# Attention's score maxima in eleven pieces instead of fifteen, the short query tile over either half of the keys

## The chip, the cores and the metric

The kernel runs on one core of one Trainium2 chip. The metric is the device time of one execution in microseconds. The median of three runs of the kernel before is 1193.37 us (1192.91 to 1196.4).

## The reference, cut to what matters

```python
def _attn_ref(q, k, v):                       # q, k, v: (4, 8, 1152, 64)
    q_pool = q.reshape(B, H, S // 2, 2, D).mean(axis=3)          # 576 queries
    scores = scale * np.matmul(q_pool, k.transpose(0, 1, 3, 2))  # 576 x 1152
    scores = scores - np.max(scores, axis=-1, keepdims=True)
    attn = np.exp(scores)
    attn = attn / (np.sum(attn, axis=-1, keepdims=True) + 1e-09)
    return np.matmul(attn, v)
```

The 32 heads (4 batches of 8) of this attention come first. A mixture of four attention experts with a top-2 gate, a low-rank mix over the sequence and a wide two-layer network follow; the change touches none of them.

## The kernel before, in words

The program has three parts, `attention`, `experts` and `mlp`. In `attention` each engine has its own list of instructions, written out by hand in Python loops over the heads; nothing plans it, and an engine goes strictly through its list. Semaphores order the engines against each other.

A head has 576 pooled queries in five tiles of 128 (`QT`; the last, the *short tile*, holds 64, `LAST`, and 64 columns of zeros) and 1152 keys in nine tiles (`KT`). Its scores are computed twice on TensorE:

- Once with the queries on the partitions, to find each query's maximum. This is the work of `max_piece`. Each of its matmuls has a tile of 128 queries as stationary operand and a third of the keys (`PIECE`, 384 columns) moving, and fills one of two banks, `maxes[0]` and `maxes[1]`, in turn. VectorE reduces the bank to one value a partition (L647) and so frees it (`max_freed`). Five tiles by three thirds make 15 pieces a head, in the order of `PIECES`.
- Once with the keys on the partitions (`score`, nine a head, four matmuls of 288 columns each: two at L392, two at L401, which also subtract the maxima, carried by the transposed `q_lo_m`). ScalarE takes the exponential (L576, `exponent`), TensorE multiplies with the values (`values`, L415), and GpSimd (`add_tiles`, L264 and L270) and VectorE (`add_late`, L668 and L673, and `sum_blocks`, L679 and L681) add the exponentials up.

The work of two heads is interleaved: while the scores of head h run, the pieces of head h + 1 fill the gaps between them. TensorE's list for a head is, before the change: score 0, pieces 0 and 1, the turning (transposing) of the last keys together with the short query tile, score 1, piece 2, score 2, piece 3, the turning of the queries of h + 2, piece 4, score 3, piece 5, the turning of the output of head h - 1 (`turn_out`, L426), piece 6, the row sums of head h - 1 (`sum_rows`, L431), piece 7, score 4, piece 8, the values of four tiles, pieces 9 and 10, score 5, piece 11, the turning of four key tiles of h + 2, piece 12, score 6, piece 13, score 7, piece 14, score 8, the turning of four more key tiles, the turning of the queries' low parts and maxima of h + 1 (`turn_q_lo_m`), the values of the other five tiles.

What holds TensorE: a piece waits until the piece two before it has been reduced; score n waits for exponential n - 2; `turn_q_lo_m` waits for the head's final maximum (`maximum`, L661), which reduces the partial ones in `part_max`. ScalarE's list has nine exponentials a head, and between them the copies out of PSUM (L546 and L547: the short query tile and the last keys; L550: four key tiles; L555: the queries; L562: low parts and maxima; L584: the output). VectorE's list: the 15 reductions of head h + 1 with `normalise(h - 1)` (L688 to L708) in front of the tenth, then L661, then the sums of head h, whose second step waits for GpSimd's additions. GpSimd's list holds, for each head, the low parts of keys and queries (L237, L246), a copy of the keys (L255), the pooling (L231) and six additions; in heads 8 to 14 it also splits the weights of the experts. The first head's maxima are computed apart (`wide_maxima`), with 1152 columns in three banks.

Of the kernel before, what the change touches and what calls it, by code (L numbers as in the profile page):

```python
# [26 lines left out]
P = 128  # L27
BANK = 512
EPS = 1e-9
MASKED = -1000000000.0  # L30

# [22 lines left out]
def attention(nc, q, k, v, x_all, x_ready, ident, ident_r, ready, ahead):  # L54
# [29 lines left out]
    PIECES = ([(t, c) for c in range(2) for t in range(QT - 1)] + [(QT - 1, 0), (QT - 1, 1)]  # L84
              + [(t, 2) for t in range(QT)])
# [18 lines left out]
    with ctx:  # L104
# [16 lines left out]
        qT = [sb(f"qT{u}", [P, WIDE], F32R) for u in range(3)]  # L121
        qTm = [sb(f"qTm{u}", [P, WIDE], F32R) for u in range(2)]
        part_max = [sb(f"part_max{u}", [P, QT, 3]) for u in range(2)]
# [30 lines left out]
        wide_reduced = sem("wide_maxima_reduced")  # L154
        padded = sem("padding_written")
# [28 lines left out]
        PADS = 8  # L184
# [133 lines left out]
        def _(pe):  # L318
# [53 lines left out]
            def max_piece(h, at):  # L372
                u, (t, c) = h % 2, PIECES[at]
                n = max_no(h, at)
                if at == 0:
                    pe.wait_ge(qa_copied, h + 1)
                for first, name in (((0, 0), "ka"), ((0, 1), "kb"), ((QT - 1, 0), "kc")):
                    if (t, c) == first:
                        pe.wait_ge(turn_freed, keys_before[name, h] + 1)
                if n >= 2:  # L380
                    pe.wait_ge(max_freed[n % 2], n // 2)
                nc.tensor.matmul(maxes[n % 2][:, 0:PIECE], qT[h % 3][:, t * P:(t + 1) * P],  # L382
                                 kT[u][:, c * PIECE:(c + 1) * PIECE], start=True, stop=True
                                 ).then_inc(max_filled, 1)
# [63 lines left out]
            for h in range(HEADS - 1):  # L448
# [17 lines left out]
                maxima(5, 6)  # L466
                if h > 0:
                    turn_out(h - 1)
                maxima(6, 7)
                if h > 0:  # L470
                    sum_rows(h - 1)
                maxima(7, 8)
                score(h, 4)
                maxima(8, 9)
                values(h, range(EARLY))
                maxima(9, 11)
                score(h, 5)
                maxima(11, 12)
                if more2:
                    turn_keys(h + 2, "ka", range(0, 4))  # L480
                maxima(12, 13)
                score(h, 6)
                maxima(13, 14)
                score(h, 7)
                maxima(14, 15)
# [38 lines left out]
        def _(act):  # L524
# [17 lines left out]
            def copy_keys(h, name):  # L542
                u = h % 2
                act.wait_ge(turned, turn_no[name, h] + 1)
                if name == "kc":
                    nc.scalar.activation(qT[h % 3][:, 4 * P:WIDE], turn[:, P:2 * P], ACT.Copy)  # L546
                    ins = nc.scalar.activation(kT[u][:, 8 * P:S], turn[:, 0:P], ACT.Copy)  # L547
                else:
                    at = 0 if name == "ka" else 4 * P
                    ins = nc.scalar.activation(kT[u][:, at:at + 4 * P], turn[:, :], ACT.Copy)  # L550
                ins.then_inc(turn_freed, 1)
# [91 lines left out]
        def _(dve):  # L643
            def max_piece(h, at):
                u, (t, c), n = h % 2, PIECES[at], max_no(h, at)
                dve.wait_ge(max_filled, n + 1)
                nc.vector.tensor_reduce(part_max[u][:, t, c:c + 1], maxes[n % 2][:, 0:PIECE],  # L647
                                        AX.X, ALU.max).then_inc(max_freed[n % 2], 1)

            def wide_maxima(t):  # L650
                dve.wait_ge(wide_filled, t + 1)
                nc.vector.tensor_reduce(part_max[0][:, t, :], wide(t), AX.X, ALU.max
                                        ).then_inc(wide_reduced, 1)

            def maximum(h):
# [3 lines left out]
                else:  # L659
                    dve.wait_ge(max_freed[n % 2], n // 2 + 1)  # L660
# [55 lines left out]
            nc.vector.memset(oT[:, HALF + SHIFT:3 * P], 0.0).then_inc(padded, 1)  # L716
            nc.vector.memset(group_sums[:, SQ // BLOCK:], 0.0).then_inc(padded, 1)
# [17 lines left out]
            for h in range(HEADS - 1):  # L735
                for at in range(len(PIECES)):
                    if at == 9 and h > 0:
# [1123 lines left out]
```

## Time and profile before

| | us |
|---|---|
| median of three runs | 1193.37 |
| the profiled execution, its own time | 1195.76 |
| its span, first to last instruction | 1194.0 |
| PE busy | 1135.8 |
| DVE busy | 651.6 |
| ACT busy | 543.9 |
| POOL busy | 523.4 |
| L647, 465 reductions of the pieces, DVE | 250.6 |
| L382, 465 matmuls of the pieces, PE | 166.0 |

The profile is one execution. PE is TensorE's matmuls, PEld its weight loads, DVE VectorE, ACT ScalarE, POOL GpSimd. A matmul's record is longer than the time it keeps the array, since successive matmuls overlap; the distance from one start to the next is what it costs. The heads fill the span from about 20 to 507 us, the experts follow to about 780, and the wide network runs to the end.

### The profile page before, as it was taken

The page shows a single profiled execution, that of the slowest core. Times are in us where ns is not written, and L with a number is a line of the kernel's source. Part 1 is how long each engine was busy: PE and PEld are TensorE (multiplying, and loading weights), DVE is VectorE, ACT ScalarE, POOL GpSimd, SP SyncE. Part 2 cuts the span into 40 slices and gives each one's busy share as a digit, 9 for nine tenths or more (in the row PEclk, how much of TensorE's full clock was granted, in tenths as well). Part 3 has the DMA queues.
Part 4 walks back from the last instruction along what each step waited for, and adds up shares of the span by engine and source line. Part 5 has one row for each costly group of instructions (what it writes and reads, how often), then busy time and mean ns, then how long its engine had stood idle before and what let it go on. Part 6 is the DMA issues. An engine that isn't in the chain of part 4 may idle for free. (4 is left out here: it accounts for less than half of the span.)

```text
span 1194.0 us, 19539 instructions
## 1 busy us (share of the span) xinstructions
PE 1135.8 (95%) x7232; PEld 951.8 (80%) x7232; DVE 651.6 (55%) x1370; ACT 543.9 (46%) x1131; POOL 523.4 (44%) x560
## 2 busy tenths in 40 slices
PE   6999999989999999997899999789999999999998
PEld 5777777777777778786777777489898989899896
DVE  5888877877888888866556565553121212122120
ACT  4666666556666666546565656633110201111110
POOL 6888899998888888734333333300000000000000
PEclk9999999999999999998999999999999999999999
DMA  8222111221111221002001010142100001010000
GB/s 205 61 60 61 56 46 51 60 60 46 51 55 60 60 60 41 22 27 115 2 1 41 1 45 24 40 146 62 53 1 27 27 1 53 0 53 0 27 1 27
DMA packets 47559, 54.56 MB, mean 46 GB/s; under 512 B 10992, under 2 KB 29424, under 8 KB 46960
## 3 DMA queue, kind: packets, MB, share of 16 engines
q1 hardware_dynamic: 46864, 53.12, 14.4%
q8 instruction: 53, 0.87, 0.3%
q10 hardware_dynamic: 608, 0.30, 0.1%
q14 instruction: 34, 0.28, 0.1%
HBM read 43.97 MB, written 9.44 MB: 45 GB/s over the span
## 5 line engine op out<-in xcount | busy, mean ns | idle before, releaser
L647 DVE TENSOR_REDUCE part_max<-psA 128x1 f32<-128x384 f32 x465 | 250.6, 556 | 59.4 <-PE psA L382 36.7
L576 ACT ACTIVATE pT<-psA 128x576 f32<-128x576 f32 x288 | 187.9, 653 | 165.5 <-PE psA L401 156.4
L270 POOL TENSOR_TENSOR pT<-pT 128x576 f32<-128x576 f32 x157 | 225.3, 1435 | 26.2 <-ACT pT L576 4.3
L382 PE MATMUL psA<-kT,qT 128*128 128x384 f32 x465 | 166.0, 379 | 11.5 <-DVE part_max L647 11.1
L415 PE MATMUL psA<-pT,v_raw 128*64 128x288 f32 x1152 | 153.8, 412 | 0.0
L1770 ACT ACTIVATE hid_hi<-psC 128x384 fp32r<-128x384 f32 x96 | 47.2, 492 | 198.7 <-PE psC L1695 198.6
L392 PE MATMUL psA<-qT,kT 128*128 128x288 f32 x576 | 132.2, 311 | 0.0
L1789 DVE SCALAR_TENSOR_TENSOR hid_lo<-psC,hid_hi 128x384 fp32r<-128x384 f32 x96 | 53.5, 558 | 137.9 <-ACT hid_hi L1770 137.9
L401 PE MATMUL psA<-qTm,kT 128*128 128x288 f32 x576 | 123.0, 295 | 0.5 <-ACT qTm L562 0.5
L415 PEld LDWEIGHTS psA<-pT,v_raw 128*64 128x64 f32 x1152 | 77.0, 136 | 53.2 <-issue 6.4
L1711 PE MATMUL psC<-w_hi,hid_hi 128*128 128x512 f32 x288 | 113.5, 394 | 0.0
L392 PEld LDWEIGHTS psA<-qT,kT 128*128 128x128 f32 x576 | 98.4, 189 | 18.4 <-issue 14.0
L382 PEld LDWEIGHTS psA<-kT,qT 128*128 128x128 f32 x465 | 83.7, 189 | 36.5 <-DVE part_max L647 19.4
L1711 PE MATMUL psC<-w_hi,hid_lo 128*128 128x512 f32 x288 | 112.3, 390 | 0.0
L1711 PE MATMUL psC<-w_lo,hid_hi 128*128 128x512 f32 x288 | 112.2, 389 | 0.0
L401 PEld LDWEIGHTS psA<-qTm,kT 128*128 128x128 f32 x576 | 92.3, 188 | 0.7 <-issue 0.7
L1695 PE MATMUL psC<-uT_hi,w_hi 128*128 128x384 f32 x384 | 82.5, 337 | 1.7 <-DVE uT_lo L44 1.7
L1147 POOL TENSOR_SCALAR moe_probs<-moe_probs,moe_sum_inv,gate 128x128 f32<-128x128 f32 (+4 forms) x80 | 53.7, 671 | 66.0 <-DVE moe_sum_inv L1520 61.8
L1695 PE MATMUL psC<-uT_hi,w_lo 128*128 128x384 f32 x384 | 82.4, 337 | 0.0
L1695 PE MATMUL psC<-uT_lo,w_hi 128*128 128x384 f32 x384 | 82.4, 337 | 0.0
L1410 ACT ACTIVATE moe_probs<-psB,moe_neg_max 128x128 f32<-128x128 f32 (+4 forms) x80 | 45.6, 570 | 65.4 <-DVE moe_neg_max L1533 64.7
L1695 PEld LDWEIGHTS psC<-uT_hi,w_hi 128*128 128x128 f32 x384 | 68.1, 188 | 2.4 <-DVE uT_lo L44 2.0
(165 smaller groups left out, 1948.2 us busy)
## 6 DMA issues: line engine op xcount, KB each, us to landing
k_raw<-in_k SPq DMA_DIRECT2D x32, 288.0 KB, 2.9
v_raw<-in_v SPq DMA_DIRECT2D x32, 288.0 KB, 2.8
q_raw<-in_q SPq DMA_DIRECT2D x31, 256.0 KB, 3.3
w_raw<-in_moe_w_ch SPq DMA_DIRECT2D x1, 4096.0 KB, 12.3
u_rows<-x_all SPq DMA_DIRECT2D x16, 256.0 KB, 2.0
w_raw<-in_moe_w_ch SPq DMA_DIRECT2D x16, 256.0 KB, 2.6
u_first<-u_rows SPq DMA_DIRECT2D x3, 768.0 KB, 4.5
u_second<-u_rows SPq DMA_DIRECT2D x3, 768.0 KB, 4.7
```

Of the source, the lines that this page charges most:

```text
L270: nc.gpsimd.tensor_tensor(pT[:, KT, :], pT[:, KT, :], pT[:, j, :], ALU.add).then_inc(part_summed, 1)
L382: nc.tensor.matmul(maxes[n % 2][:, 0:PIECE], qT[h % 3][:, t * P:(t + 1) * P], kT[u][:, c * PIECE:(c + 1) * PIECE], start=True, stop=True). ...
L392: nc.tensor.matmul(out[:, half, 0:HALF], kT[u][:, j * P:(j + 1) * P], qT[h % 3][:, half * HALF:(half + 1) * HALF], start=True, stop=False)
L401: mm = nc.tensor.matmul(out[:, half, 0:HALF], kT1[u][:, j * P:(j + 1) * P], qTm[u][:, half * HALF:(half + 1) * HALF], start=False, stop=True)
L415: mm = nc.tensor.matmul(o_bank[half * D:(half + 1) * D, at:at + HALF], v_raw[u][:, j, :], pT[:, j, half * HALF:(half + 1) * HALF], start=( ...
L576: nc.scalar.activation(pT[:, j, :].rearrange("p (a c) -> p a c", a=2), scores[n % 2][:, :, 0:HALF], ACT.Exp, scale=0.5 * float(D) ** -0.5) ...
L647: nc.vector.tensor_reduce(part_max[u][:, t, c:c + 1], maxes[n % 2][:, 0:PIECE], AX.X, ALU.max).then_inc(max_freed[n % 2], 1)
L1147: nc.gpsimd.tensor_scalar(p, p, sum_inv[0:rows, e, i:i + 1], gate[b % 2][0:rows, i, e:e + 1], ALU.mult, ALU.mult).then_inc(scaled, 1)
L1695: mm = nc.tensor.matmul(up[f % 4], w1_s[w][:, k, f * P:(f + 1) * P], uT[x][:, k, :], start=((w, x, k) == (*PARTS3[0], 0)), stop=((w, x, k) ...
L1711: mm = nc.tensor.matmul(down[t], hid[h][:, f, t * P:(t + 1) * P], w2_s[w][:, f, :], start=(n == 0), stop=(n == 3 * FC - 1))
L1770: nc.scalar.activation(hid[0][:, f, :], up[f % 4], ACT.Relu).then_inc(up_hi, 1)
L1789: nc.vector.scalar_tensor_tensor(hid[1][:, f, :], up[f % 4], 0.0, hid[0][:, f, :].bitcast(F32), ALU.max, ALU.subtract).then_inc(up_lo, 1)
```

## The change

- `PIECES` becomes eleven. Four pieces ("a") are one of the full query tiles by the first 512 keys, four ("b") by the next 512. One ("c") puts the last 128 keys of all four full tiles side by side in one bank, with four matmuls of 128 columns. Two ("half") are for the short tile.
- The short tile's 64 queries stand twice behind the others in `qT`, now 768 columns wide: columns 512 to 575 and 640 to 703, with zeros at 576 to 639 and 704 to 767. The window 512 to 639 so has the queries in its lower 64 columns, and the window 576 to 703 in its upper 64. A half piece accumulates two matmuls: lower window by the first 576 keys and upper window by the second 576; partitions 0 to 63 then hold the queries' scores over one half of the keys and partitions 64 to 127 over the other. The 576 columns are cut into 512 and 64, one piece each.
- `part_max` has four columns a tile; unused ones hold -3e38, written once at the start by two further memsets. `maximum` first copies the short tile's two partial maxima from partitions 64 to 127 to partitions 0 to 63, waits for that (`halves_moved`), and then reduces 128 x 20 instead of 128 x 15 values.
- ScalarE's copy of the short tile (L546) writes it twice.
- TensorE's order: after score 3 come piece 5, score 4, pieces 6 and 7, then the turning of the last output and its row sums, then the values of four tiles, piece 8, score 5, piece 9, the turning of four key tiles, score 6, piece 10, score 7, score 8. `normalise` comes in front of the ninth reduction.

```diff
--- before.py
+++ after.py
@@ -28,6 +28,7 @@
 BANK = 512
 EPS = 1e-9
 MASKED = -1000000000.0
+LOWEST = -3.0e38
 
 
 def ceil_div(a, b):
@@ -81,8 +82,13 @@
     v_v = v.rearrange("b h (p j) d -> p (b h) j d", p=P)
     q_v = q.rearrange("b h (r two) d -> (b h) r (two d)", two=2)
 
-    PIECES = ([(t, c) for c in range(2) for t in range(QT - 1)] + [(QT - 1, 0), (QT - 1, 1)]
-              + [(t, 2) for t in range(QT)])
+
+
+
+    PIECES = ([("a", t) for t in range(QT - 1)] + [("b", t) for t in range(QT - 1)]
+              + [("c", None), ("half", 0), ("half", 1)])
+    HALF_KEYS = S // 2
+
 
     TURN_USES = [("ka", 0), ("kb", 0), ("kc", 0), ("ka", 1), ("kb", 1)]
     for h in range(HEADS):
@@ -118,9 +124,9 @@
 
         kT = [sb(f"kT{u}", [P, S], F32R) for u in range(2)]
         kT1 = [sb(f"kT1{u}", [P, S], F32R) for u in range(2)]
-        qT = [sb(f"qT{u}", [P, WIDE], F32R) for u in range(3)]
+        qT = [sb(f"qT{u}", [P, WIDE + P], F32R) for u in range(3)]
         qTm = [sb(f"qTm{u}", [P, WIDE], F32R) for u in range(2)]
-        part_max = [sb(f"part_max{u}", [P, QT, 3]) for u in range(2)]
+        part_max = [sb(f"part_max{u}", [P, QT, 4]) for u in range(2)]
         pT = sb("pT", [P, KT + 1, SQ])
         p_sum = sb("p_sum", [P, SQ])
         p_turned = sb("p_turned", [P, SQ])
@@ -152,6 +158,7 @@
         q_padded = sem("queries_padded")
         wide_filled = sem("wide_maxima_filled")
         wide_reduced = sem("wide_maxima_reduced")
+        halves_moved = sem("halves_moved")
         padded = sem("padding_written")
         k1_zeroed = sem("k1_rows_zeroed")
         pooled = sem("pooled")
@@ -181,7 +188,7 @@
         x_full = sem("full_tiles_written")
         block = ctx.enter_context(nc.Block())
 
-        PADS = 8
+        PADS = 10
 
         def load_q(eng, h):
             u = h % 2
@@ -370,18 +377,32 @@
                 mm.then_inc(wide_filled, 1)
 
             def max_piece(h, at):
-                u, (t, c) = h % 2, PIECES[at]
+                u, (kind, t) = h % 2, PIECES[at]
                 n = max_no(h, at)
+                out, q, k = maxes[n % 2], qT[h % 3], kT[u]
                 if at == 0:
                     pe.wait_ge(qa_copied, h + 1)
-                for first, name in (((0, 0), "ka"), ((0, 1), "kb"), ((QT - 1, 0), "kc")):
-                    if (t, c) == first:
+                for first, name in ((("a", 0), "ka"), (("b", 0), "kb"), (("c", None), "kc")):
+                    if PIECES[at] == first:
                         pe.wait_ge(turn_freed, keys_before[name, h] + 1)
                 if n >= 2:
                     pe.wait_ge(max_freed[n % 2], n // 2)
-                nc.tensor.matmul(maxes[n % 2][:, 0:PIECE], qT[h % 3][:, t * P:(t + 1) * P],
-                                 kT[u][:, c * PIECE:(c + 1) * PIECE], start=True, stop=True
-                                 ).then_inc(max_filled, 1)
+                if kind == "half":
+                    a, z = ((0, BANK), (BANK, HALF_KEYS))[t]
+
+                    parts = [(out[:, 0:z - a], q[:, c:c + P],
+                              k[:, m * HALF_KEYS + a:m * HALF_KEYS + z])
+                             for m, c in enumerate(((QT - 1) * P, SQ))]
+                elif kind == "c":
+                    parts = [(out[:, t * P:(t + 1) * P], q[:, t * P:(t + 1) * P], k[:, 2 * BANK:S])
+                             for t in range(QT - 1)]
+                else:
+                    at = 0 if kind == "a" else BANK
+                    parts = [(out, q[:, t * P:(t + 1) * P], k[:, at:at + BANK])]
+                for m, (to, queries, keys) in enumerate(parts):
+                    mm = nc.tensor.matmul(to, queries, keys, start=kind != "half" or m == 0,
+                                          stop=kind != "half" or m == 1)
+                mm.then_inc(max_filled, 1)
 
             def score(h, j):
                 u, n = h % 2, h * KT + j
@@ -464,25 +485,21 @@
                 maxima(4, 5)
                 score(h, 3)
                 maxima(5, 6)
+                score(h, 4)
+                maxima(6, 8)
+
                 if h > 0:
                     turn_out(h - 1)
-                maxima(6, 7)
-                if h > 0:
                     sum_rows(h - 1)
-                maxima(7, 8)
-                score(h, 4)
+                values(h, range(EARLY))
                 maxima(8, 9)
-                values(h, range(EARLY))
-                maxima(9, 11)
                 score(h, 5)
-                maxima(11, 12)
+                maxima(9, 10)
                 if more2:
                     turn_keys(h + 2, "ka", range(0, 4))
-                maxima(12, 13)
                 score(h, 6)
-                maxima(13, 14)
+                maxima(10, 11)
                 score(h, 7)
-                maxima(14, 15)
                 score(h, 8)
                 if more2:
                     turn_keys(h + 2, "kb", range(4, 8))
@@ -543,7 +560,9 @@
                 u = h % 2
                 act.wait_ge(turned, turn_no[name, h] + 1)
                 if name == "kc":
-                    nc.scalar.activation(qT[h % 3][:, 4 * P:WIDE], turn[:, P:2 * P], ACT.Copy)
+                    nc.scalar.activation(
+                        qT[h % 3][:, 4 * P:].rearrange("p (n c) -> p n c", c=P),
+                        turn[:, P:2 * P].unsqueeze(1).to_broadcast([P, 2, P]), ACT.Copy)
                     ins = nc.scalar.activation(kT[u][:, 8 * P:S], turn[:, 0:P], ACT.Copy)
                 else:
                     at = 0 if name == "ka" else 4 * P
@@ -642,14 +661,23 @@
         @block.vector
         def _(dve):
             def max_piece(h, at):
-                u, (t, c), n = h % 2, PIECES[at], max_no(h, at)
+                u, (kind, t), n = h % 2, PIECES[at], max_no(h, at)
+                src = maxes[n % 2]
                 dve.wait_ge(max_filled, n + 1)
-                nc.vector.tensor_reduce(part_max[u][:, t, c:c + 1], maxes[n % 2][:, 0:PIECE],
-                                        AX.X, ALU.max).then_inc(max_freed[n % 2], 1)
+                if kind == "half":
+                    to = part_max[u][:, QT - 1, t:t + 1]
+                    src = src[:, 0:BANK if t == 0 else HALF_KEYS - BANK]
+                elif kind == "c":
+                    to = part_max[u][:, 0:QT - 1, 2]
+                    src = src.rearrange("p (t k) -> p t k", k=P)
+                else:
+                    c = 0 if kind == "a" else 1
+                    to = part_max[u][:, t, c:c + 1]
+                nc.vector.tensor_reduce(to, src, AX.X, ALU.max).then_inc(max_freed[n % 2], 1)
 
             def wide_maxima(t):
                 dve.wait_ge(wide_filled, t + 1)
-                nc.vector.tensor_reduce(part_max[0][:, t, :], wide(t), AX.X, ALU.max
+                nc.vector.tensor_reduce(part_max[0][:, t, 0:3], wide(t), AX.X, ALU.max
                                         ).then_inc(wide_reduced, 1)
 
             def maximum(h):
@@ -657,7 +685,13 @@
                 if h == 0:
                     dve.wait_ge(wide_reduced, QT)
                 else:
-                    dve.wait_ge(max_freed[n % 2], n // 2 + 1)
+                    for m in (n - 1, n):
+                        dve.wait_ge(max_freed[m % 2], m // 2 + 1)
+
+                    nc.vector.tensor_copy(part_max[u][0:LAST, QT - 1, 2:4],
+                                          part_max[u][LAST:P, QT - 1, 0:2]
+                                          ).then_inc(halves_moved, 1)
+                    dve.wait_ge(halves_moved, h)
                 nc.vector.tensor_reduce(q_lo_m[u][:, :, D], part_max[u][:, :, :], AX.X, ALU.max,
                                         negate=True).then_inc(m_ready, 1)
 
@@ -714,6 +748,8 @@
             for u in range(2):
                 nc.vector.memset(q_lo_m[u][:, :, D:2 * D].bitcast(F32), 0.0).then_inc(padded, 1)
             nc.vector.memset(oT[:, HALF + SHIFT:3 * P], 0.0).then_inc(padded, 1)
+            nc.vector.memset(part_max[0][:, :, 3:4], LOWEST).then_inc(padded, 1)
+            nc.vector.memset(part_max[1][:, :, 2:4], LOWEST).then_inc(padded, 1)
             nc.vector.memset(group_sums[:, SQ // BLOCK:], 0.0).then_inc(padded, 1)
             dve.wait_ge(made, 2)
             by_group = ident[:, :].rearrange("p (g i) -> p g i", i=BLOCK)
@@ -734,7 +770,7 @@
             maximum(0)
             for h in range(HEADS - 1):
                 for at in range(len(PIECES)):
-                    if at == 9 and h > 0:
+                    if at == 8 and h > 0:
                         normalise(h - 1)
                     max_piece(h + 1, at)
                 maximum(h + 1)
```

## Rows read from the trace of the kernel before

**Rows 1.** The page, part 1: busy time, share of the span, instructions.
```profile
PE 1135.8 (95%) x7232; PEld 951.8 (80%) x7232; DVE 651.6 (55%) x1370; ACT 543.9 (46%) x1131; POOL 523.4 (44%) x560
```
**Rows 2.** L661 in three stretches: durations in ns; first, last start in us.
```profile
L661 DVE TENSOR_REDUCE q_lo_m<-part_max x9: 170/171/171, 50.2 to 172.9; 128x5 fp32r<-128x15 f32 x9
...
L661 DVE TENSOR_REDUCE q_lo_m<-part_max x8: 170/172/173, 172.9 to 292.3; 128x5 fp32r<-128x15 f32 x8
...
L661 DVE TENSOR_REDUCE q_lo_m<-part_max x15: 170/171/172, 292.3 to 506.6; 128x5 fp32r<-128x15 f32 x15
```
**Rows 3.** Windows: length, busy time of PE, PEld, DVE, ACT, POOL, clock, DMA.
```profile
189.20:205.80 16.60, 15.53 (x115) 12.17 (x113) 12.94 (x27) 10.18 (x19) 15.80 (x15) 1.00 0.19 55
307.60:322.90 15.30, 15.29 (x114) 12.12 (x113) 12.65 (x26) 10.18 (x19) 12.69 (x11) 1.00 0.20 59
```
**Rows 4.** Waits from 189.2 to 222.3 us: total, times, longest.
```profile
DVE p_sum L673 <- POOL pT L270: 2.6, 2, 1.3
```
**Rows 5.** Timeline of PE, 311.0 to 326.4 us: start, length, engine, line.
```profile
311.60 0.52 PE L382 MATMUL psA<-kT,qT 128*128 128x384 f32 x2
311.95 0.22 PE L328 MATMUL psA<-ident_r,k_parts 128*128 128x128 f32 x1
312.01 0.22 PE L328 MATMUL psA<-ident_r,q_hi 128*128 128x128 f32 x1
...
312.66 0.36 PE L382 MATMUL psA<-kT,qT 128*128 128x384 f32 x1
312.87 0.42 PE L392 MATMUL psA<-qT,kT 128*128 128x288 f32 x2
...
314.81 0.49 PE L426 MATMUL psA<-ident,oT 128*128 128x128 f32 x3
...
316.70 2.16 PE L415 MATMUL psA<-pT,v_raw 128*64 128x288 f32 x16
318.80 0.62 PE L382 MATMUL psA<-kT,qT 128*128 128x384 f32 x2
...
321.25 0.33 PE L382 MATMUL psA<-kT,qT 128*128 128x384 f32 x1
...
322.79 0.45 PE L328 MATMUL psA<-ident_r,k_parts 128*128 128x128 f32 x4
323.19 0.60 PE L328 MATMUL psA<-ident_r,q_lo_m 128*128 128x128 f32 x5
```
**Rows 6.** The chain that ended last, in order of time: start, length, line.
```profile
820.21 10.92 PE psC L1711 x48
...
853.86 33.29 PE psC L1695 x192
```
**Rows 7.** Timelines of PEld at 568 us and of PE at 566 us.
```profile
568.41 0.30 PEld L1235 LDWEIGHTS psB<-moe_kT,moe_qT 128*128 128x128 f32 x2
...
565.76 0.48 PE L1235 MATMUL psB<-moe_kT,moe_qT 128*64 128x512 f32 x3
```
**Rows 8.** Groups by line, 0 to 60 us: busy us, mean ns, idle before.
```profile
L647 DVE TENSOR_REDUCE part_max<-psA 128x1 f32<-128x384 f32 x39 | 21.0, 556 | 7.8 <-PE psA L382 5.6
...
L652 DVE TENSOR_REDUCE part_max<-psA 128x3 f32<-128x1152 f32 x5 | 6.6, 1354 | 5.4 <-PE psA L367 5.4
```
**Rows 9.** Timeline of DVE, 310.9 to 326.4 us.
```profile
322.92 0.17 DVE L661 TENSOR_REDUCE q_lo_m<-part_max 128x5 fp32r<-128x15 f32 x1
```
**Rows 10.** Groups by line, 310.9 to 326.2 us, ACT.
```profile
L576 ACT ACTIVATE pT<-psA 128x576 f32<-128x576 f32 x9 | 5.9, 652 | 4.8 <-PE psA L401 4.5
...
L550 ACT ACTIVATE kT<-psA 128x512 fp32r<-128x512 f32 x2 | 1.2, 602 | 0.0
...
L546 ACT ACTIVATE qT<-psA 128x128 fp32r<-128x128 f32 x1 | 0.3, 271 | 0.0
```
**Rows 11.** Timeline of POOL, 310.9 to 326.4 us.
```profile
310.31 1.42 POOL L237 TENSOR_TENSOR k_parts<-k_raw,k_parts 128x576 fp32r<-128x576 f32 x1 [1.61 <-ACT k_parts L530]
```
**Rows 12.** Timeline of DVE, 0 to 14 us.
```profile
5.59 0.49 DVE L231 TENSOR_TENSOR q_pool<-q_raw 128x320 f32<-128x320 f32 x1 [2.57 <-DMA q_raw<-in_q]
```

## The prediction, made before the changed kernel was run

> **What bounds the kernel now.** I read the page first [rows 1]: the reader is to see PE busy for 95% of the span, the mark of a kernel whose order is set on TensorE, and DVE at 55%. Since an average hides stages, the next view is the spacing of one instruction that runs once a head, the final maximum of L661 [rows 2]. Its first and last starts give (172.9 − 50.2) / 8 = 15.34 us a head, then (292.3 − 172.9) / 7 = 17.06 us for seven heads, then (506.6 − 292.3) / 14 = 15.31 us. So there are 22 light heads and 7 heavy ones. The heavy ones are those in which GpSimd also splits the experts' weights: in a head of 16.60 us it is busy for 15.80 [rows 3], VectorE's late sum waits for it, 1.3 us at the longest [rows 4], and everything behind that sum, the next head's maxima too, waits along. POOL is the bound there, and the change takes nothing from POOL. The light heads I walk on PE [rows 5], start to start, because the duration of a matmul carries a pipeline tail. Nearly every start is the predecessor's price away; what PE loses to others is little. So a light head is bound by PE's issue, with VectorE close behind in the stretches of dense pieces.
>
> **The change part by part.**
>
> *Price of the pieces.* The long stages give the price: 192 matmuls of 384 columns in 33.29 us, 0.173 each, and 48 of 512 in 10.92, 0.228 each [rows 6]. The 15 pieces cost 15 × 0.173 = 2.60 us a head. The new ones stream just as many columns (8 × 512 + 4 × 128 + 2 × 512 + 2 × 64 = 5760 = 15 × 384). Ten of them are long: 10 × 0.228 = 2.28. Six are short, and for those the price is not the columns: two weight loads of 128 columns in front of 128-column matmuls span 0.30 us with 0.19 for one, so they start 0.11 apart [rows 7], twice what 128 columns take (128 × (0.228 − 0.173) / 128 = 0.055). Six times 0.11 is 0.66; together 2.94, or 0.34 more than before. Bounds for a short one: 0.055 (streaming) and 0.19 (a load that overlaps nothing); I take 0.11, since that row has the same shape on both sides. That they would run at a quarter of the rate I leave out: in the row of 565.76 a 512-column matmul and two of 64 columns end 0.48 us after the first start [rows 7]; 0.23 of that is the long one and 0.19 the tail that any matmul's record carries (0.36 at 312.66 for a piece of 0.173 [rows 5]), which leaves 0.03 each, where 256 columns' worth would be 0.11.
>
> *Price of a reduction.* 384 elements take 0.556 us and 1152 take 1.354 [rows 8], so 1.04 ns an element and 512 take 0.556 + 128 × 0.00104 = 0.69. Bounds: 0.556 (nothing added) and 0.741 (in proportion). The view of four times 128 has as many elements and the same price. DVE a head: before 15 × 0.556 = 8.34; after 10 × 0.69 + 64 elements at 0.22 = 7.12. The copy between partitions is not in the trace; small DVE operations take 0.17 (L661) [rows 9], bounds 0 and 0.5 with its wait. VectorE thus does about 1 us less, but it is not what bounds the head; the gain can only appear where PE waits for a bank.
>
> *The head, segment by segment* (light head, PE starts of [rows 5]; scores cost 4 × 0.133, the 288-column price by the slope above).
> (a) The first two pieces: 311.60 to 311.95 is 0.35; two long ones 0.46. **+0.10.**
> (b) The third waits for the first's bank. Before, 312.66 to 312.87, 0.21: 0.04 over its price, so the bank came free just about in time. After, the fill is 0.05 and the reduction 0.13 longer, while PE arrives 0.10 later: some 0.12 late, 0.34 in all. **+0.13** (bounds 0.02 if the reduction doesn't grow, 0.18).
> (c) The next three lie between scores, as before, each 0.055 longer. **+0.16.**
> (d) From 314.81 to 316.70, 1.89 us, PE turned the output (0.25), summed its rows and ran three pieces and a score. After: score 0.53, two long pieces 0.46, turns 0.25, row sums 0.21 (two weight loads at 0.11) = 1.45. But the two pieces now stand side by side behind one score: the second needs the bank of the piece before that score, filled 0.39 after its start (0.34 for a short wait-free one, and 0.05), reduced in 0.69, with 0.09 for the two semaphores (my estimate from the timelines' spacing: 0.04 from fill to reduction, 0.05 from there to a weight load), so 1.17 after it. PE is there after 0.23 + 0.53 + 0.23 = 0.99, and its weight load, which had been fetched ahead, shows for 0.11: a wait of 0.30. 1.75 in all, **−0.14** (bounds −0.44 without the wait, −0.09). Behind that waiting piece stand the turns, the row sums and the first values, so all of them move with it.
> (e) From 318.80 to 322.79, 3.99 us. After: the one piece of four short ones behind the values, 0.11 exposed load + 4 × 0.11 = 0.55; score 0.53; first half 0.46; keys turned 0.29; score behind turns 0.59 (312.01 to 312.66 is a turn of 0.06 and such a score). The rest, from the end of score 6 to the end of score 8, is not PE's to set: score 8 needs exp 6. Before it took 322.79 − 321.25 = 1.54, 0.20 to exp 6, its 0.65 [rows 10], 0.05 and the late score's 0.64. The two pieces (0.35) that stood in it were free; now one short pair (0.22) stands there, and 1.54 remains. Total 3.96. **−0.04** (−0.38 to +0.4 with the bounds of the short ones).
> (f) From 322.79 to 323.19 four turns took 0.40, because the low parts' turn waited for the maximum that starts at 322.92 [rows 9]. After, the last reduction ends 0.22 after a small fill, before score 8; copy, semaphore and maximum end about 0.7 us before they are needed. That is the cover of the added copy and its wait: behind it on DVE stands only that maximum, for which PE's q_lo turns wait. 0.28. **−0.12.**
> Sum: 0.10 + 0.13 + 0.16 − 0.14 − 0.04 − 0.12 = **+0.09 us a light head**, 22 × 0.09 = 2.0 us. Heavy heads: 0, POOL's loop holds no changed instruction.
>
> *At nothing.* ScalarE writes the short tile twice: 128 columns more in an activation of 0.27 (L546) [rows 10], between nothing and 0.27 longer, I take 0.1 (ScalarE needs 0.33 more for 384 columns more, as the key copy of L550 there shows). It stands in front of exp 1, whose score's successor but one comes later than that, and POOL's key copy behind it has 1.61 us of idle time later in the head [rows 11]. The output's turn and normalisation come 0.1 to 0.2 us later and are wanted, by the turning of keys, more than 1 us after. Score 4 and its exp come 0.8 earlier, score 5 0.4 later; POOL's fifth addition then just meets exp 5, and its idle time takes a slip. Two more memsets at the start stand in front of 2.57 us in which DVE waits for the queries [rows 12]; uncovered they would cost 0.1 each, once.
>
> *A rule against the row.* For the price of a short matmul the row of [rows 7] says 0.11. The Trainium skill ("TensorE: Matmul & The Clock Gate", section "Back-to-back issue gap") gives columns / 2.4 GHz plus 2.5 ns for a lone matmul. By it all pieces, old and new, would cost 2.44 us, the 0.34 would be nothing, and the sum would turn; the case is the first rival below. The trace does not agree in [rows 6]: 384 columns cost 0.173 there against 0.1625 by the rule.
>
> **The rivals.**
> *Short ones at streaming price* (0.055). For: turns of 128 columns start 0.06 apart, 311.95 to 312.01 [rows 5]. Against: their weight loads are of another kind, 0.14 against 0.19. It gives back 6 × 0.055 = 0.33: 0.09 − 0.33 = −0.24 a head, −5.3 us, 1188.1. Chance 0.11.
> *VectorE's relief counts.* If PE's waits in (b) and (d) vanish, as they would with a reduction of 0.56 or if I have misplaced the bank's return, 0.11 + 0.30 go: −0.32 a head, −7.0 us, 1186.4. For: PE did wait for banks before. Against: pieces are longer and stand closer. Chance 0.12.
> *Bare weight loads* (slower). Place: the six short matmuls; price 0.19 − 0.11 = 0.08 each, 0.48 a head, with my sum 0.57, 12.5 us, 1205.9. It decides once loads stand more than 0.12 apart. For: the accumulating pairs of two query windows change their weights each time. Against: the pair of [rows 7]. Chance 0.12.
> *VectorE sets the pace* (slower). A reduction of 0.74 adds 0.05 to each of the two waits; the score behind also slips: 0.19 a head, 4.2 us, 1197.6. Chance 0.17.
>
> **How the numbers follow.** My case has 0.48. The profiled execution took 1195.76 us around a span of 1194.0, 2.4 above the median of 1193.37 shown; the sum adds 2.0: 1197.8 on its own base, **1195.4** on the median's. 0.3% of it, 3.6 us, is what I take a measurement to tell from no change. My case and what surrounds it lie within that: same 0.48; both faster rivals 0.23; both slower ones 0.29. The likeliest case's own range is 1192 to 1199. With the bounds above the range runs from 1187 to 1203, which leaves out the ends of the second and the third rival.
>
> **What would show it.** Light heads 15.3 to 15.5 us apart at L661's successor, heavy ones unchanged near 17; long pieces 0.23 apart, the four short ones 0.11; a wait of 0.3 at the eighth piece and 0.1 at the third; score 8 still waiting for exp 6; no wait at the q_lo turns; reductions of 0.69. I am wrong if light heads come below 15.15 (one of the first two rivals; the distance of the short ones tells which) or above 15.5, or if the heavy heads move by more than 0.1.

## The result and the profile after

| | before | changed |
|---|---|---|
| median of 9 runs, us | 1194.94 | 1199.9 |
| profiled execution: own time, span, us | 1195.76, 1194.0 | 1198.34, 1196.6 |
| light heads, from final maximum to final maximum, us | 15.32 | 15.56 |
| DVE busy, us | 651.6 | 621.7 |

The changed kernel is slower: the ratio of its runs to those of the kernel before is 1.0038, with a 95% interval of 1.0026 to 1.0049. I had forecast 1195.4 on a median of 1193.37, a ratio of 1.0017; the time lies in my range and on the side of the sum. But the loss is 2.5 times what the sum said (5.0 us of the medians, 2.0 forecast), and I gave the largest chance to "no change that can be told", and it can be told.

The page of the changed kernel, the lines on engines and on the pieces. They answer to [rows 1]:
```profile
PE 1138.0 (95%) x7263; PEld 943.0 (79%) x7263; DVE 621.7 (52%) x1279; ACT 546.6 (46%) x1131; POOL 521.8 (44%) x560
...
L676 DVE TENSOR_REDUCE part_max<-psA 128x1 f32<-128x512 f32 (+2 forms) x341 | 212.4, 646 | 74.0 <-PE psA L403 67.5
```
VectorE does 30 us less in all, and its idle time in front of the reductions is 74.0 us, 67.5 of it waiting for PE. What was taken off VectorE did not bound the kernel.

The final maximum of the changed kernel (L695), in the three stretches of [rows 2]:
```profile
L695 DVE TENSOR_REDUCE q_lo_m<-part_max x9: 175/175/176, 50.4 to 174.7; 128x5 fp32r<-128x20 f32 x9
...
L695 DVE TENSOR_REDUCE q_lo_m<-part_max x8: 175/175/176, 174.7 to 293.1; 128x5 fp32r<-128x20 f32 x8
...
L695 DVE TENSOR_REDUCE q_lo_m<-part_max x15: 175/176/177, 293.1 to 511.0; 128x5 fp32r<-128x20 f32 x15
```
Light heads: (174.7 − 50.4) / 8 = 15.54 and (511.0 − 293.1) / 14 = 15.56 us, 0.20 and 0.26 more than before; 22 of them make 5.2 us. The seven heavy ones take 118.4 us against 119.4. A window of one heavy head shows that POOL still fills it (15.77 of 16.50 us, the fifth pair of numbers):
```profile
191.30:207.80 16.50, 15.66 (x113) 11.94 (x113) 11.72 (x23) 10.26 (x20) 15.77 (x14) 1.00 0.19 55
```
So the last final maximum comes 4.4 us later, and the loss is made in the light heads alone.

One light head of the changed kernel, PE by start, as in [rows 5]; here it begins at 328.11:
```profile
328.74 0.62 PE L403 MATMUL psA<-kT,qT 128*128 128x512 f32 x2
329.20 0.22 PE L335 MATMUL psA<-ident_r,k_parts 128*128 128x128 f32 x1
...
329.92 0.50 PE L403 MATMUL psA<-kT,qT 128*128 128x512 f32 x1
330.26 0.43 PE L413 MATMUL psA<-qT,kT 128*128 128x288 f32 x2
...
332.93 0.91 PE L403 MATMUL psA<-kT,qT 128*128 128x512 f32 x2
333.68 0.49 PE L447 MATMUL psA<-ident,oT 128*128 128x128 f32 x3
334.00 0.30 PE L452 MATMUL psA<-group_sums,all_groups 128*128 128x20 f32 x2
334.23 2.16 PE L436 MATMUL psA<-pT,v_raw 128*64 128x288 f32 x16
336.32 0.66 PE L403 MATMUL psA<-kT,qT 128*128 128x128 f32 x4
336.82 0.48 PE L413 MATMUL psA<-qT,kT 128*128 128x288 f32 x2
...
340.30 0.47 PE L335 MATMUL psA<-ident_r,k_parts 128*128 128x128 f32 x4
340.61 0.58 PE L335 MATMUL psA<-ident_r,q_lo_m 128*128 128x128 f32 x5
```
Read the differences of starts. The first two pieces take 0.46 (329.20 − 328.74). The third takes 0.34. The seventh and eighth take 0.75 side by side, 0.29 over their price of 0.46; the eighth's weight load, at 333.34, had waited 0.35 us for a reduction. The four short matmuls of piece c take 0.50. From 336.32 to 340.30 it is 3.98.

The weight loads of piece c, and the one in front of score 8 with what it waited for (PEld):
```profile
336.32 0.52 PEld L403 LDWEIGHTS psA<-kT,qT 128*128 128x128 f32 x4 [0.44 <-issue]
...
339.66 0.30 PEld L413 LDWEIGHTS psA<-qT,kT 128*128 128x128 f32 x2 [0.23 <-ACT pT L595]
```
Four loads span 0.52 with 0.19 for the last, so they start 0.11 apart. Score 8 still waits for an exponential.

The end of the maxima on DVE, answering to [rows 9]:
```profile
339.43 0.35 DVE L691 COPY part_max<-part_max 64x2 f32<-64x2 f32 x1
339.82 0.17 DVE L695 TENSOR_REDUCE q_lo_m<-part_max 128x5 fp32r<-128x20 f32 x1
```
The final maximum ends at 339.99, 0.6 before the turn at 340.61 that needs it.

### The profile page after: what moved, and what is told of

The parts are those of the page before. It is cut to its first block and busy times, and to the rows that moved or that the text cites. A ratio compares the mean times of both kernels' runs of the same rounds, so it can differ in the third digit from the quotient of the medians.

```text
span 1196.6 us, 19541 instructions
## 1 busy us (share of the span) xinstructions
PE 1138.0 (95%) x7263; PEld 943.0 (79%) x7263; DVE 621.7 (52%) x1279; ACT 546.6 (46%) x1131; POOL 521.8 (44%) x560
## 5 line engine op out<-in xcount | busy, mean ns | idle before, releaser
L676 DVE TENSOR_REDUCE part_max<-psA 128x1 f32<-128x512 f32 (+2 forms) x341 | 212.4, 646 | 74.0 <-PE psA L403 67.5
L403 PE MATMUL psA<-kT,qT 128*128 128x512 f32 (+1 forms) x496 | 150.4, 364 | 10.2 <-DVE part_max L676 9.5
L413 PE MATMUL psA<-qT,kT 128*128 128x288 f32 x576 | 138.6, 322 | 0.0
L413 PEld LDWEIGHTS psA<-qT,kT 128*128 128x128 f32 x576 | 93.5, 189 | 25.2 <-issue 14.0
L403 PEld LDWEIGHTS psA<-kT,qT 128*128 128x128 f32 x496 | 80.7, 188 | 37.5 <-DVE part_max L676 22.0
```

Source lines behind the costliest of these rows:

```text
L403: mm = nc.tensor.matmul(to, queries, keys, start=kind != "half" or m == 0, stop=kind != "half" or m == 1)
L413: nc.tensor.matmul(out[:, half, 0:HALF], kT[u][:, j * P:(j + 1) * P], qT[h % 3][:, half * HALF:(half + 1) * HALF], start=True, stop=False)
L676: nc.vector.tensor_reduce(to, src, AX.X, ALU.max).then_inc(max_freed[n % 2], 1)
```

## The experiments

The light heads' spacing tells more than a median here: the two light stretches of one trace agree to 0.03 us a head, while whole executions of one kernel lie up to 7.5 us apart. Each run below is read by it first. These are the final maxima of the kernels in the second light stretch, first and last start. The number behind x, less one, is the count of heads. Before and changed, then the four of the first set:
```profile
L661 DVE TENSOR_REDUCE q_lo_m<-part_max x12: 170/171/171, 307.6 to 476.1; 128x5 fp32r<-128x15 f32 x12
```
```profile
L695 DVE TENSOR_REDUCE q_lo_m<-part_max x12: 175/176/176, 308.6 to 479.9; 128x5 fp32r<-128x20 f32 x12
```
```profile
L696 DVE TENSOR_REDUCE q_lo_m<-part_max x13: 175/176/178, 308.3 to 492.5; 128x5 fp32r<-128x20 f32 x13
```
```profile
L694 DVE TENSOR_REDUCE q_lo_m<-part_max x13: 175/176/177, 312.4 to 496.5; 128x5 fp32r<-128x20 f32 x13
```
```profile
L696 DVE TENSOR_REDUCE q_lo_m<-part_max x13: 175/175/178, 307.8 to 491.6; 128x5 fp32r<-128x20 f32 x13
```
```profile
L658 DVE TENSOR_REDUCE q_lo_m<-part_max x13: 170/171/171, 312.5 to 502.5; 128x5 fp32r<-128x15 f32 x13
```
That is 15.32, 15.57, 15.35, 15.34, 15.32 and 15.83 us a head.

**The eighth piece behind the row sums.**
```diff
-                maxima(6, 8)
+                maxima(6, 7)
                 if h > 0:
                     turn_out(h - 1)
                     sum_rows(h - 1)
+                maxima(7, 8)
                 values(h, range(EARLY))
```


> The changed kernel with one edit in TensorE's order: the eighth piece comes behind the turning of the last output and its row sums instead of in front of them; the work is the same. In the changed kernel's light head the seventh and eighth piece take 0.75 us side by side where their price is 0.46. My theory (0.29 of it is the wait for the bank of the sixth piece, the rest of the head does not need that time): the wait goes, one weight load behind the row sums shows for up to 0.1; light heads 15.37 to 15.42 us apart instead of 15.57, and 4 us less in all. Rival (the wait only moves to the next piece, or the DVE work behind comes later and delays the keys' turning): light heads stay at 15.5 to 15.6.

Measured: 15.35 us a light head; ratio to the kernel before 1.0021 (1.0004 to 1.0038). PE in that place:
```profile
332.16 0.39 PE L403 MATMUL psA<-kT,qT 128*128 128x512 f32 x1
332.39 0.49 PE L447 MATMUL psA<-ident,oT 128*128 128x128 f32 x3
332.71 0.30 PE L452 MATMUL psA<-group_sums,all_groups 128*128 128x20 f32 x2
332.86 0.48 PE L403 MATMUL psA<-kT,qT 128*128 128x512 f32 x1
333.26 2.16 PE L436 MATMUL psA<-pT,v_raw 128*64 128x288 f32 x16
```
From the seventh piece to the values it is 1.10 instead of 1.30, and the head gains 0.22. The wait for the bank was real and did not move elsewhere. Of its 0.29 some 0.1 came back in the same place: turns, row sums and the two pieces take 1.10 where their prices (0.32, 0.23 and 0.46) give 1.01.

**Piece c as one matmul.**
```diff
-                    parts = [(out[:, t * P:(t + 1) * P], q[:, t * P:(t + 1) * P], k[:, 2 * BANK:S])
-                             for t in range(QT - 1)]
+                    parts = [(out, q[:, 0:P], k[:, S - BANK:S])]
```


> The changed kernel with piece c as a single matmul of 512 columns in place of four of 128 (it leaves out the last 128 keys of the full tiles' maxima: the bank holds the first tile's scores over the last 512 keys instead); VectorE reduces as many elements. If short matmuls cost their weight load (0.11 each, my price), the segment falls from 0.50 to about 0.34 (0.23 and the load that shows behind the values) and the score behind it from 0.59 to 0.53: light heads 15.57 - 0.2 = 15.35 us apart. If they cost their columns alone, nothing changes: 15.57.

Measured: 15.34; ratio 1.0015 (0.9998 to 1.0031). PE from the piece to the end of the score behind it:
```profile
339.61 0.50 PE L402 MATMUL psA<-kT,qT 128*128 128x512 f32 x1
339.95 0.42 PE L412 MATMUL psA<-qT,kT 128*128 128x288 f32 x2
...
340.48 0.62 PE L402 MATMUL psA<-kT,qT 128*128 128x512 f32 x2
```
The piece takes 0.34 and the score 0.53, as written down. With as many columns and three weight loads fewer the head is 0.23 us shorter: a short matmul costs its load.

**Reductions of 384 instead of 512.**
```diff
                     to = part_max[u][:, t, c:c + 1]
+                    src = src[:, 0:384]
```


> The changed kernel with VectorE reducing only the first 384 of the 512 columns of each a and b piece (it leaves 128 keys a piece out of the maxima); TensorE's work is unchanged. If the longer reduction makes the waits at the third piece (0.10 over its price) and at the eighth (0.29 over), both shrink by 0.13: light heads 15.57 - 0.25 = 15.3 us apart (15.33 if the third piece had only 0.10 to give). Rival (the waits are TensorE's own: the load of weights, the fill's tail): light heads stay within 0.05 of 15.57.

Measured: 15.32; ratio 1.0012 (1.0 to 1.0024). The two pieces side by side, from 331.50 to the turns at 332.12, take 0.62 instead of 0.75:
```profile
331.50 0.79 PE L403 MATMUL psA<-kT,qT 128*128 128x512 f32 x2
332.12 0.49 PE L447 MATMUL psA<-ident,oT 128*128 128x128 f32 x3
...
343.95 0.39 PE L403 MATMUL psA<-kT,qT 128*128 128x512 f32 x1
344.18 0.43 PE L413 MATMUL psA<-qT,kT 128*128 128x288 f32 x2
```
The third piece takes 0.23, its price, instead of 0.34, and the head is 0.25 shorter, the two together. Both waits follow the length of the reduction.

**The new order with the old fifteen pieces.**
```diff
                 maxima(5, 6)
-                if h > 0:
-                    turn_out(h - 1)
-                maxima(6, 7)
-                if h > 0:
-                    sum_rows(h - 1)
-                maxima(7, 8)
                 score(h, 4)
-                maxima(8, 9)
+                maxima(6, 9)
+                if h > 0:
+                    turn_out(h - 1)
+                    sum_rows(h - 1)
                 values(h, range(EARLY))
```


> The kernel before with only TensorE's order changed as in the change: score 4 behind the sixth piece, then pieces seven, eight and nine side by side, then the turning of the last output, the row sums and the values. Fifteen pieces of 384 columns stay. My theory (side-by-side pieces wait for banks: each needs the reduction two before it, 0.34 + 0.56 + 0.09 = 0.99 us after that one's start): the eighth waits about 0.15 and the ninth about 0.3, less 0.2 for weight loads no longer shown in front of single pieces; light heads 15.32 + 0.2 to 0.35 = 15.5 to 15.7. Rival (the order is neutral and the change's loss is all in the pieces' lengths): 15.32.

Measured: 15.83; ratio 1.0092 (1.0073 to 1.0112). The direction was right and the size was not:
```profile
351.88 0.72 PE L382 MATMUL psA<-kT,qT 128*128 128x384 f32 x2
352.96 0.41 PE L382 MATMUL psA<-kT,qT 128*128 128x384 f32 x1 [0.36 <-DVE part_max L644]
353.21 0.49 PE L426 MATMUL psA<-ident,oT 128*128 128x128 f32 x3
353.54 0.30 PE L431 MATMUL psA<-group_sums,all_groups 128*128 128x20 f32 x2
```
Three pieces take 1.33 us where their price is 0.52: 0.8 of waits. From the first to the third it is 1.08, 0.73 over the price of two, where I had written 0.15 and 0.3; the round of a bank was right to 0.1 (0.99), and the waits I drew from it were not. The order with fifteen pieces costs twice what the whole change costs. With eleven pieces only two stand there.

The final maxima of the second set, in its order: both edits, keys turned before score 8, halves of 288, no copy; and of the last kernel below.
```profile
L695 DVE TENSOR_REDUCE q_lo_m<-part_max x13: 175/177/179, 306.8 to 488.6; 128x5 fp32r<-128x20 f32 x13
```
```profile
L696 DVE TENSOR_REDUCE q_lo_m<-part_max x13: 175/176/177, 305.4 to 486.7; 128x5 fp32r<-128x20 f32 x13
```
```profile
L690 DVE TENSOR_REDUCE q_lo_m<-part_max x13: 175/175/177, 306.3 to 487.5; 128x5 fp32r<-128x20 f32 x13
```
```profile
L691 DVE TENSOR_REDUCE q_lo_m<-part_max x12: 175/175/177, 310.0 to 481.2; 128x5 fp32r<-128x20 f32 x12
```
```profile
L689 DVE TENSOR_REDUCE q_lo_m<-part_max x13: 175/176/177, 305.6 to 486.4; 128x5 fp32r<-128x20 f32 x13
```
That is 15.15, 15.11, 15.10, 15.56 and 15.07 us a head.

**Both edits** (the first two above together).

> The two edits of the runs before together in the changed kernel: the eighth piece behind the row sums, and piece c as a single matmul of 512 columns (it leaves out the last 128 keys of the full tiles' maxima). Each alone brought light heads from 15.57 to 15.35 us. If they remove two separate costs, they add up: 15.14 (between 15.1 and 15.2). Rival: some third resource holds a head at about 15.3, which would also explain why three different edits all ended between 15.31 and 15.36; then 15.3 again.

Measured: 15.15; ratio 0.9979 (0.9964 to 0.9994). Two gains of 0.22 and 0.23 come to 0.42 together. No third resource stands at 15.3.

**Keys turned in front of score 8** (with the eighth piece behind the row sums).
```diff
                 score(h, 7)
-                score(h, 8)
                 if more2:
                     turn_keys(h + 2, "kb", range(4, 8))
+                score(h, 8)
```


> The changed kernel with the eighth piece behind the row sums and with the turning of the second four key tiles in front of score 8 instead of behind it; complete. In the changed kernel score 8 waits for exponential 6 (from the end of score 6 to the end of score 8 it is 1.54 us, 0.25 of it a wait), and the turning costs 0.30 behind it. My theory: the turning fits into that wait but for 0.1, so light heads fall from 15.35 to 15.15 (15.1 to 15.2). Rival (the end of score 8 is not set by the exponential but by TensorE's own issue): 15.35, the turning only changes its place.

Measured: 15.11; ratio 0.9982 (0.9971 to 0.9993). Of the 0.31 that the turning took behind score 8, 0.24 is gained. This kernel leaves nothing out and is 0.2% faster than the one before.

**Halves of 288, thirds of 384.** From the changed kernel; TensorE's order is that of the kernel before, with one piece fewer behind the first values.
```diff
+    PIECES = ([(0, t) for t in range(QT - 1)] + [(1, t) for t in range(2)]
+              + [("half", 0), ("half", 1)] + [(1, t) for t in range(2, QT - 1)]
+              + [(2, t) for t in range(QT - 1)])
...
-                    a, z = ((0, BANK), (BANK, HALF_KEYS))[t]
+                    a, z = t * HALF_KEYS // 2, (t + 1) * HALF_KEYS // 2
...
-                    if at == 8 and h > 0:
-                        normalise(h - 1)
+                    if at == 9:
+                        if h > 0:
+                            normalise(h - 1)
+                        ...
+                        nc.vector.tensor_copy(part_max[u][0:LAST, QT - 1, 2:4],
+                                              part_max[u][LAST:P, QT - 1, 0:2]
+                                              ).then_inc(halves_moved, 1)
```


> Fourteen pieces: the four full tiles as before by thirds of 384 columns (twelve pieces), only the short tile by halves of the keys, in two pieces of two accumulating matmuls of 288 columns each; the copy of the upper halves stands in front of the tenth reduction, away from the end of the head; TensorE's order as before with the last single gap closed. Complete. No short matmul, TensorE's price 12 x 0.173 + 4 x 0.133 = 2.61 against 2.60 before and 2.93 in the change; VectorE 12 x 0.556 + 2 x 0.456 + the copy's 0.35 = 7.9 against 8.34. My theory: light heads at or a little under 15.32, 15.15 to 15.3, since only waits of 0.1 here and there are there to be won. Rival (accumulating pairs with two windows carry a cost of their own): 15.4 or more.

Measured: 15.10; ratio 0.9956 (0.9936 to 0.9977), and in a second set of runs, against the same kernel before, 0.9947 (0.9929 to 0.9965). For the second set I expected:

> The kernel of fourteen pieces once more, beside the one above on the same chip: light heads 15.10 us apart, 0.995 to 0.996 of the kernel before.

Its light heads lie 15.14 apart (304.5 to 486.2, twelve heads), one of them 15.6 and the others 15.10. So two executions of one kernel differ by 0.04 in this average.

PE around the half pieces, of which each is two matmuls of 288 columns:
```profile
343.71 0.49 PE L445 MATMUL psA<-ident,oT 128*128 128x128 f32 x3
343.95 0.51 PE L401 MATMUL psA<-kT,qT 128*128 128x288 f32 x2
344.30 0.29 PE L450 MATMUL psA<-group_sums,all_groups 128*128 128x20 f32 x2
344.52 0.54 PE L401 MATMUL psA<-kT,qT 128*128 128x288 f32 x2
```
The first pair takes 0.35 and the second 0.38, 0.27 of each by price and the rest the load behind the turns and the row sums. What is gained stands between the first values and the turning behind score 8:
```profile
332.68 0.44 PE L401 MATMUL psA<-kT,qT 128*128 128x384 f32 x1
...
336.28 0.46 PE L336 MATMUL psA<-ident_r,k_parts 128*128 128x128 f32 x4
```
That is 3.60 us against 3.99 (318.80 to 322.79 in [rows 5]), with one piece fewer. Of this 0.39 some 0.17 goes back, in the half pieces and in the turning behind score 8 (0.48, 336.28 to 336.76, against 0.40). By the ratio this is the fastest kernel of the study, together with the last one below: the halves of the keys for the short tile alone, without short matmuls. No run takes its 0.39 apart.

**The copy taken away.**
```diff
-                    nc.vector.tensor_copy(part_max[u][0:LAST, QT - 1, 2:4],
-                                          part_max[u][LAST:P, QT - 1, 0:2]
-                                          ).then_inc(halves_moved, 1)
-                    dve.wait_ge(halves_moved, h)
```


> The changed kernel without the copy of the short tile's partial maxima between partitions and without its wait (it leaves out half of the keys in the short tile's maxima). I hold the copy (0.35 us by the trace, twice what I took) to be covered: VectorE's final maximum ends 0.6 us before TensorE needs it. Light heads 15.57 us apart as in the changed kernel. Rival (it delays the late sums and, through them, the next head's first pieces): 15.4 or less.

Measured: 15.56 us a head, as with it (15.57); one run of 1199.4 us. The copy is covered.

**Fourteen pieces, keys turned in front of score 8.** The fourteen-piece kernel with the last piece moved up:
```diff
-                maxima(12, 13)
+                maxima(12, 14)
                 score(h, 7)
-                maxima(13, 14)
-                score(h, 8)
                 if more2:
                     turn_keys(h + 2, "kb", range(4, 8))
+                score(h, 8)
```


> The kernel of fourteen pieces (light heads 15.10 us) with two places changed at the end of a head: the last piece goes in front of score 7, beside the thirteenth, and the turning of the second four key tiles comes in front of score 8 instead of behind it. Complete. In the kernel of fourteen pieces the turning behind score 8 takes 0.48 us, 0.18 of it a wait for the final maximum, and score 8 still waits for exponential 6. My theory: the maximum comes before it is needed and the turning fills what the exponential leaves, so that 0.48 falls away and 0.3 come back in front of score 8: light heads 14.9 to 15.0. Rival (the two side-by-side pieces wait for their bank by as much): 15.1 or more.

Measured: 15.07; ratio 0.9958 (0.9942 to 0.9975). A miss: 0.03 gained of the 0.1 to 0.2 expected, which is less than the 0.04 between the two executions of the kernel it is compared with. The rival was right about the place:
```profile
349.36 0.73 PE L401 MATMUL psA<-kT,qT 128*128 128x384 f32 x2
349.93 0.42 PE L411 MATMUL psA<-qT,kT 128*128 128x288 f32 x2
```
Two pieces side by side take 0.57 where their price is 0.35. The same wait as in the change, made anew.

## Why the prediction was right in its parts, and where it was not

Light head, PE's starts of both profiles, us:

| step | predicted | measured |
|---|---|---|
| (a) two pieces | +0.10 | +0.11 |
| (b) third piece | +0.13 | +0.13 |
| (c) three pieces between scores | +0.16 | +0.16, and 0.04 in the scores and turns around them |
| (d) seventh piece to the values | −0.14 | −0.05 |
| (e) piece c to score 8 | −0.04 | −0.01 |
| (f) turns behind score 8 | −0.12 | −0.09 |
| values, score 0 and turns of q_lo | 0 | −0.05 |
| sum | +0.09 | +0.24 (by the spacing +0.25) |

*The mechanism held.* The forecast named short matmuls at 0.11, reductions of 0.69 (688 ns on average for 512 elements), a wait of 0.3 at the eighth piece and 0.1 at the third, score 8 set by exponential 6, heavy heads held by POOL, and the copy covered; each stands so in the trace. The runs show four of these by taking them away: the eighth piece's wait, the price of piece c, the reduction's length behind both waits, the copy. What I had put at nothing stayed there: ScalarE's double write takes 0.38 instead of 0.27 and the two memsets 0.06 and 0.07, and no wait in the trace stands behind them.

*Two of my own signs of being wrong came true all the same.* Light heads are above 15.5 (15.54 and 15.56), and the heavy ones moved by 0.14 each, not by less than 0.1. That the time lies in my range says little, since the range is 16 us wide.

*The step that failed is (d).* It gives 0.09 of the 0.16 that a head is off. The wait in it was right (0.75 measured for the two pieces, 0.76 predicted), but I carried the three turns over at 0.25. That was their price with a piece behind them. In the trace of before they take 0.24 and the piece behind them 0.26, 0.09 over its own price, starting from 314.81 in [rows 5]:
```profile
315.05 0.42 PE L382 MATMUL psA<-kT,qT 128*128 128x384 f32 x1
315.31 0.29 PE L431 MATMUL psA<-group_sums,all_groups 128*128 128x20 f32 x2
```
With the row sums behind, the turns take 0.32 (333.68 to 334.00), also in the run with the eighth piece moved (332.39 to 332.71), and 0.33 in the one with fifteen pieces (353.21 to 353.54). In the fourteen-piece kernel, where a piece follows again, they take 0.24 (343.71 to 343.95). As I read these rows, one load of 128 columns shows behind the short turns whatever follows them; I had booked it for the piece and dropped it with the piece. The row sums add 0.02 (0.23 for 0.21). The rest, some 0.07, is in terms of 0.01 to 0.04 of both signs, as the table has them; no run tells what they are.

*The sum to the whole.* The light heads make 5.2 us and the first maximum comes 0.2 later; less 1.0 in the heavy stretch, the last maximum comes 4.4 later. The two profiled executions differ by less, 2.6 us, since all that follows the heads took 1.8 us less in the changed kernel's (685.6 against 687.4), for which I know no reason; the medians differ by 5.0. In the heavy stretch four of the seven heads take 66.3 us before and 66.2 changed, so POOL's hold on them is as I said. The one microsecond lies in the last three: 19.3, 16.6 and 17.2 before, 17.9, 19.1 and 15.2 changed. The head of 19.3:
```profile
239.20:258.50 19.30, 16.87 (x114) 13.55 (x112) 12.75 (x27) 10.22 (x19) 18.36 (x16) 0.91 0.16 46
```
There PE stood idle once for 2.43 us, up to 246.81, and from about 248 to 252 its granted clock was 0.50, the lower of its two levels. In the changed kernel PE stood idle twice in this stretch, for 2.16 and 2.22 us, and the clock stayed at 1.00. What the lower clock cost there no run tells.

*The rivals.* "Short ones at streaming price" fell with the single matmul in piece c: the same columns, 0.23 us less a head. By the rule of the Trainium skill that stood beside it ("TensorE: Matmul & The Clock Gate", section "Back-to-back issue gap") the two forms differ by 0.01, an estimate from its figures; the measurement decides against it where each matmul brings its own load. The same page's section "LDWEIGHTS (loading the stationary operand)" gives columns / 1.2 GHz, 0.107 for 128, and with that the trace agrees (0.11). "VectorE's relief counts" fell too: 30 us less work on VectorE, and light heads 0.25 us longer. "Bare weight loads" fell with loads 0.11 apart. "VectorE sets the pace" had the waits in the right places and comes nearest in time (0.19 a head, 4.2 us), but by a price that does not hold: a reduction takes 0.69, not 0.74.

*The chances.* My error over a head was 0.16 us, and 0.16 us by 22 heads is 3.5 us, nearly all of the 3.6 us that I had set between "no change" and "slower". A sum of small terms of both signs, repeated 22 times, deserved a flatter spread: the likeliest case's own range of 1192 to 1199 already reached across.

## What to carry to other kernels

When matmuls of equal total length are cut anew, count their weight loads as well as their columns: here a stationary operand of 128 columns needs 0.11 us, and a matmul that streams for less, 0.055 at 128 columns, pays the load instead. Pieces that pass through two banks in turn belong apart in the order, each behind some other work as long as fill, reduction and semaphores less one piece; side by side they cost the difference. And relief on an engine that is not the bound is worth only what it removes from the bound's waits, which the spacing of starts shows before anything is built.

## Not expected of the hardware

- The copy of 64 partitions by 2 elements from the upper to the lower half took 0.35 us (median) in the changed kernel and 0.65 on average in the fourteen-piece one, where it follows the normalisation, against 0.18 for a reduction of 128 by 20. No run tells why.
- Order alone, with the old pieces and no other change, cost 0.51 us a head and 0.9% of the whole, twice the change itself.
